# The high parts of q and k: two transfers on POOL's queue instead of two engine copies

## The reference

```python
scores = scale * np.matmul(q, k.transpose(0, 1, 3, 2))
cum = np.cumsum(np.maximum(s, 0.0), axis=-1)
bias = -(cum[:, :, :, None] - cum[:, :, None, :])
scores = np.where(causal, -1000000000.0, scores + np.minimum(bias, 0.0))
attn = softmax(scores)                       # with 1e-9 added to the sum
x = (attn @ v) with heads side by side       # 2304 x 512
x = np.maximum(np.maximum(x @ w1, x @ w2), x @ w3) @ w_out      # inner width 768
y = ((x @ w_a) * (x @ w_b)) @ w_out2                            # inner width 1536
```

## Time and profile before

| | us |
|---|---|
| median of 3 runs | 982.70 (982.25 to 982.79) |
| the profiled execution, device time | 982.89 |
| its span, first to last instruction | 981.1 |
| PE busy | 941.4 (96%) |
| weight loads busy | 859.0 (88%) |
| DVE busy | 465.4 (47%) |
| ACT busy | 406.4 (41%) |
| POOL busy | 215.7 (22%) |
| granted clock of TensorE over the span | 1.00 |

### The profile page before, as it was taken

The page is one execution under the profiler, slowest core; times in us unless marked ns, Lnnn a source line. Parts: engine busy times, 40 slices in busy tenths (PEclk is TensorE's granted clock), DMA queues, the critical chain, the costliest instruction groups (busy, mean ns, idle before and its releaser), DMA issues.

```text
span 981.1 us, 15222 instructions
## 1 busy us (share of the span) xinstructions
PE 941.4 (96%) x5776; PEld 859.0 (88%) x5776; DVE 465.4 (47%) x1054; ACT 406.4 (41%) x912; POOL 215.7 (22%) x309
## 2 busy tenths in 40 slices
PE   3789899999999999999999999999999999999998
PEld 2588899999999999999999888888888888888898
DVE  6789788877666577563233433221122112211212
ACT  4778677676655556543223432211121112111211
POOL 6868554453432423410000000000000000000000
PEclk9999999999999999999999999999999999999999
DMA  3644322222121221100032332200020001000100
GB/s 115 225 147 141 96 85 71 68 75 77 63 79 39 84 65 53 48 2 27 16 130 88 101 97 92 77 9 1 0 82 5 1 1 65 1 0 1 43 1 22
DMA packets 29240, 58.74 MB, mean 60 GB/s; under 512 B 3184, under 2 KB 15568, under 8 KB 29136
## 3 DMA queue, kind: packets, MB, share of 16 engines
q1 hardware_dynamic: 29168, 57.77, 18.4%
HBM read 47.82 MB, written 9.88 MB: 59 GB/s over the span
## 4 chain that ended last, share of the span: by engine, by line
PE 93%; issue 2%; DVE 1%; DMA 1%; ACT 1%; POOL 1%; SPq 0%; DVEq 0%; POOLq 0%; ACTq 0%
PE bank L1175 30%; PE bank L1047 23%; PE bank L1190 15%; PE bank L1067 8%; PE bank L998 6%; PE bank L1028 6%; PE bank L1014 5%; DMA qk_st<-cum_row 1%; DVE soft L790 0%; DMA qk_raw<-in_qk 0%; POOL soft L486 0%; ACT soft L536 0%; SPq L383 0%; DMA x_raw<-in_s 0%; POOL qk_st L477 0%
## 5 line engine op out<-in xcount | busy, mean ns | idle before, releaser
L957 DVE TENSOR_TENSOR g_raw<-bank,a_sb 128x512 f32<-128x512 f32 (+1 forms) x60 | 38.3, 638 | 298.5 <-PE bank L1175 298.5
L1047 PE MATMUL bank<-xs_hi,w_hi 128*128 128x256 f32 (+1 forms) x576 | 174.0, 302 | 1.9 <-DVE xs_lo L811 1.2
L1047 PE MATMUL bank<-xs_hi,w_lo 128*128 128x256 f32 (+1 forms) x576 | 170.7, 296 | 0.0
L1047 PE MATMUL bank<-xs_lo,w_hi 128*128 128x256 f32 (+1 forms) x576 | 170.6, 296 | 0.0
L486 POOL TENSOR_SCALAR soft<-soft,rden 128x576 f32<-128x576 f32 (+4 forms) x160 | 102.1, 657 | 216.6 <-DVE rden L776 216.6
L1175 PE MATMUL bank<-y_hi,w2b_hi 128*128 128x512 f32 (+1 forms) x360 | 132.4, 368 | 0.0
L1175 PE MATMUL bank<-y_lo,w2b_hi 128*128 128x512 f32 (+1 forms) x360 | 132.4, 368 | 0.0
L1175 PE MATMUL bank<-y_hi,w2b_lo 128*128 128x512 f32 (+1 forms) x360 | 132.4, 368 | 0.0
L1047 PEld LDWEIGHTS bank<-xs_hi,w_hi 128*128 128x128 f32 x576 | 109.4, 190 | 3.4 <-DVE xs_lo L811 1.4
L702 ACT ACTIVATE a_sb<-bank 128x512 f32<-128x512 f32 (+1 forms) x60 | 33.3, 555 | 188.5 <-PE bank L1175 188.5
L536 ACT ACTIVATE soft<-soft,neg_max 64x576 f32<-64x576 f32 (+4 forms) x160 | 96.0, 600 | 35.4 <-DVE neg_max L790 34.2
(11 more groups left out here) (84 smaller groups left out, 1825.7 us busy)
## 6 DMA issues: line engine op xcount, KB each, us to landing
qk_raw<-in_qk SPq DMA_DIRECT2D x32, 576.0 KB, 3.8
w_raw<-in_w SPq DMA_DIRECT2D x40, 384.0 KB, 3.6
v_raw<-in_v SPq DMA_DIRECT2D x32, 160.0 KB, 2.2
y_raw<-y_dram SPq DMA_DIRECT2D x4, 1024.0 KB, 5.5
outT<-o_stage SPq DMA_DIRECT2D x16, 256.0 KB, 2.1
qk_raw<-in_qk SPq DMA_DIRECT2D x8, 256.0 KB, 3.2
y_dram<-m_tmp SPq DMA_DIRECT2D x8, 160.0 KB, 1.8
y_dram<-h_raw SPq DMA_DIRECT2D x8, 160.0 KB, 1.8
```

Of the source, the lines that this page charges most:

```text
L1047: ins = nc.tensor.matmul(up_ps[g][:, 0:width1(c)], up1_w(w, f, g, kc), x[:, kc, 0:width1(c)], start=(kc == 0 and at == 0), stop=(kc == KC ...
```

## The change

POOL's copy `upper` and ACT's copy `lower` are removed with their semaphores. In the place of `upper` POOL's queue issues two transfers per job (`round_qk`), straight from the input in memory into `qk_st`: q and k for the upper half into blocks 0 and 1, and k and q for the lower half into blocks 1 and 2. The destination is float32r, so the transfer rounds. The two raise `qk_rounded[x % 2]` by 16 each. SP's load shrinks to the lower half, 64 partitions. `split_q` and `split_k` now wait for both the raw data and `qk_rounded`; the scores wait for `qk_rounded`. `round_qk(0)` and `round_qk(1)` stand at the very start of POOL's queue, ahead of the constants.

```diff
             def load_qk(x):
-                need(sp, upper_done, x - 1)
                 need(sp, qk_split, 2 * (x - 1))
-                dst, src = qk_raw[x % 2][:, :], qk[head(x), :, :]
+                dst, src = qk_raw[x % 2][DH:P, :], qk[head(x), DH:P, :]
...
         def _(pool):
+            def round_qk(x):
+
+                need(pool, score_done, TB[max(x - 1, 0)])
+                need(pool, qk_split, 2 * (x - 1))
+                cols = keys(x)
+                for p0, block in ((0, 0), (DH, 1)):
+                    nc.gpsimd.dma_start(qk_st[x % 2][p0:p0 + DH, block:block + 2, 0:cols],
+                                        qk[head(x), p0:p0 + DH, :].rearrange("p (a n) -> p a n", a=2)[:, :, 0:cols]
+                                        ).then_inc(qk_rounded[x % 2], 16)
+
+            round_qk(0)
+            round_qk(1)
             nc.gpsimd.memset(ones, 1.0).then_inc(ones_ready, 1)
...
-            upper(0)
-            upper(1)
...
                 if n != FIRST[0] - 1 and live(n + prepared(n)):
-                    upper(n + prepared(n))
+                    round_qk(n + prepared(n))
...
         def _(act):
-            def lower(x):
-
-                act.wait_ge(qk_loaded[x % 2], 16 * (x // 2 + 1))
-                need(act, score_done, TB[max(x - 1, 0)])
...
             def split_q(x):
-                dve.wait_ge(lower_done, x + 1)
+                dve.wait_ge(qk_loaded[x % 2], 16 * (x // 2 + 1))
+                dve.wait_ge(qk_rounded[x % 2], 32 * (x // 2 + 1))
...
                 if k == 0:
-                    pe.wait_ge(upper_done, n + 1)
+                    pe.wait_ge(qk_rounded[n % 2], 32 * (n // 2 + 1))
```

More of the change, by code:

```diff
@@ L270, in program @@
         v_loaded = sem("v_loaded")
-        upper_done, lower_done, qk_split = sem("upper_done"), sem("lower_done"), sem("qk_split")
+        qk_rounded = [sem("qk_rounded0"), sem("qk_rounded1")]
+        qk_split = sem("qk_split")
         v_hi_done, v_split = sem("v_hi_done"), sem("v_split")
@@ L470, in _ @@
                                     base=0, pattern=[[-1, P]], channel_multiplier=1).then_inc(ident_ready, 1)
[L472 to L479, removed]
             def normalise(n, k):
@@ L534, in exp @@
                 act.wait_ge(neg_done, TB[n] + k + 1)
+                if TB[n] + k == 0:
+                    act.wait_ge(init_done, 3)
                 i = tiles(n)[k]
@@ L578, in _ @@
             act.wait_ge(init_done, 1)
-            nc.scalar.activation(sums_eps[:, 0:1], sums[0][:, 0:1], ACT.Exp)
-            lower(0)
-            lower(1)
+            nc.scalar.activation(sums_eps[:, 0:1], sums[0][:, 0:1], ACT.Exp).then_inc(init_done, 1)
             def w1_hi_copy(piece):
@@ L596, in alone_slot @@
                 exp(n, 2)
-                if n < FIRST[0] - 1:
-                    lower(n + 2)
                 if ahead_of(n) is not None:
@@ L620, in sparse_slot @@
                     pt_hi_copy(m, 1)
-                lower(n + 1)
                 exp(n, 2)
@@ L645, in slot @@
                     x_hi(rest, KC - 1)
-                if live(n + 1):
-                    lower(n + 1)
                 if pending_row(n) is not None:
```

## The result

The changed kernel takes 1040.39 us in the median (1038.55 to 1043.68), the kernel before 982.75 us on the same chip: a ratio of 1.059 (95% interval 1.058 to 1.060), 58 us slower, where 23 us were forecast. The profiled execution took 1039.98 us, its span is 1038.2 us.

The account below looks back on a forecast made before the run. In sparse slots DVE's standstill at `split_q` was taken to be kernel time, while PE has a reserve in dense slots. Terms 12 + 5 + 2 + 4 = +23 us took 982.9 to 1006 us; 8-in-10 range 984 to 1040.

Parts of the forecast that it names:

- L: Time from POOL being free to issue until both transfers have landed; forecast 4.0 us, bounds 2.6 to 7.6 us.
- Sparse slots with w1 work: Jobs 10 to 16: DVE stalls at `split_q` where its lead is shorter than L, less some stretching; +12 us.
- Sparse slots without it: Jobs 17 to 25: leads mostly about 3.5 us, DVE stalls for the rest of L; +5.1 us.
- Dense slots: Jobs 26 to 39: shortfalls of 6.5 us, mostly covered by PE's reserve of about 0.5 us a slot; +2 us.
- Start and slots 1 to 8: Start effects cancel, then POOL's own pace of about 4.7 us a job costs 6 jobs x 0.6; +4 us.
- (b): Sign in the profile: 3.8 to 4.2 us from start of the first issue to landing of the second.
- (c): Sign: DVE idle ahead of `split_q` for a transfer into `qk_st`, 30 to 35 us in sum.
- (e): Sign at the start: first scores at about 10.8 us instead of 9.19.
- (f): Sign at the end: the last stretch, 554 us long, unchanged.
- Rival 1: Transfers hide behind the leads if L is 2.6 us or less; 981 or 979 us, not slower; chance 0.11.
- Rival 2: DVE starves POOL's transfers, L becomes 6 us; 1018 to 1065 us; chance 0.12 together with one other rival.
- Rival 3: PE leaves its upper clock level during stalls, six slots at half speed; about 1048 us; chance 0.03.

Follow-up runs that it names:

- the filler run: Changed kernel plus 24 needless products on PE ahead of `output(m)` in 12 sparse slots; 1047.52 us, ratio 1.066 to the kernel before.
- the best version: Changed kernel with jobs 0 to 9 by engine copies, jobs 10 to 39 by transfers issued early, behind `split_v(n)` for job n+2; 979.90 us, ratio 0.9974.

## Why the prediction was wrong, step by step

**What bounds the kernel** was read rightly: a stall of DVE at `split_q` comes out in the kernel's time, and reciprocal, normalise, transfers, split and reciprocal form one loop that doesn't heal. The direction, the place and the price of 20 to 25 us per microsecond of L held (24 between the lower half alone and the pair).

**L is the step that failed.** "A transfer of 144 KB lands like v's 160 KB." A half is 64 partitions of 1152 elements of 4 bytes, 288 KB; the size was halved by a slip, though the earlier trace rows give 576 KB for both halves. The 288 KB land 3.8 us after the start of their issue, not 1.0 + 1.85 = 2.85. The two are not side by side either: the second needs 4.5 us from its own start. The issue was over-priced: 0.59 and 0.53 us, not 1.0 each, and that took back 0.9 us. From the end of the second issue to its landing it is 4.0 us where 1.85 and 0.15 stood. So L = 5.1 in place of 4.0 us. The row that would have told was there: 576 KB in 3.8 us from SP's queue, and 3.8 + 1.0 us of issue is 4.8, which the prediction priced at about 1028 us.

The Trainium skill (DMA: Bandwidth & Descriptors, Rules for kernel authors) says that two transfers to disjoint halves of the partitions serialize and asks for one of 128. This trace agrees in part: the second lands 1.3 us after the first, more than the 0.6 us between their issues. The estimate of 992 us from the fit on that page was further off than the forecast; with 288 KB the fit gives an estimate of 2.7 us for a transfer, the trace shows 3.8.

**Sparse slots with w1 work**, jobs 10 to 16: +12 forecast, +19.0 measured. The seven jobs all had a lead below 4.0 us; 1.1 us more of L is 7 x 1.1 = 7.7, so the sum re-priced is 19.7.

**Sparse slots without it**, jobs 17 to 25: +5.1 forecast, +14.3 measured. Re-priced 5.1 + 9 x 1.1 = 15.0.

**Dense slots**: +2 forecast, +11.9 measured. Here too the mechanism held and L was the wrong term. At 5.1 us the leads of the 14 jobs fall short by 20.2 us in all, not by 6.5. The reserve that the prediction set against that, about 0.5 us a slot, is there. From the reciprocal to the next split the 14 slots take 22.2 us more than before. From the split to the reciprocal they take 10.3 us less, for in the kernel before DVE also waits in that stretch, for PE's scores and for ACT, and a DVE that comes late finds these ready. DVE behind the split of job 30, before and after:

```profile
286.55 0.76 DVE L790 CUSTOM_DVE_ANT_0 soft<-bank,causal 64x576 f32<-64x576 f32 x1 [1.63 <-PE bank L998]
```

```profile
337.30 0.76 DVE L780 CUSTOM_DVE_ANT_0 soft<-bank,causal 64x576 f32<-64x576 f32 x1
```

Where no such wait is left, the slot pays in full. That of job 28 takes 13.81 us in the kernel before, in the changed one 15.2:

```profile
280.18 2.78 POOL L490 TENSOR_SCALAR soft<-soft,rden 128x128 f32<-128x128 f32 x5 [9.92 <-DVE rden L766]
282.89 1.12 POOL L466 DMA_DIRECT2D qk_st<-in_qk  x2
...
295.44 2.78 POOL L490 TENSOR_SCALAR soft<-soft,rden 128x128 f32<-128x128 f32 x5 [9.96 <-DVE rden L766]
```

```profile
288.15 0.76 DVE L745 TENSOR_TENSOR qk_st<-qk_raw,qk_st 64x576 fp32r<-64x576 f32 x1 [2.52 <-DMA qk_st<-in_qk]
...
295.15 0.19 DVE L766 RECIPROCAL rden<-sums_eps 128x5 f32<-128x5 f32 x1 [0.16 <-DVE sums_eps L763]
```

From split to reciprocal DVE takes 7.0 us here in both kernels; from reciprocal to transfers issued and landed it is 0.3 + 2.7 + 5.1. That makes 15.2 with the hand-overs. Re-priced, the term is 20.2 less 14 x 0.5, 13.2 us.

**Start and slots 1 to 8**: +4 forecast, +12.4 measured. The first rows:

```profile
1.25 2.62 POOL L466 DMA_DIRECT2D qk_st<-in_qk  x4 [0.81 <-POOLq L1224]
3.86 0.60 POOL L472 MEMSET x_raw<- 32x576 f32 x1
...
11.06 1.19 PE L988 MATMUL bank<-qk_st 128*128 128x128 f32 x4 [11.06 <-DMA qk_st<-cum_row]
...
19.42 0.42 DVE L745 TENSOR_TENSOR qk_st<-qk_raw,qk_st 64x256 fp32r<-64x256 f32 x1 [5.48 <-DMA qk_st<-in_qk]
```

The memset slips to 3.86 us and the scan behind it by 0.8 us, not 1.5, but an instruction behind the scan took 1.54 us in place of 0.45, and so the first scores come at 11.06 us (10.8 forecast, 9.19 before). The rest is crowding, which the prediction had not priced. Around 13 to 19 us the DMA engines are nearly full, among other things with the cumulated sums and the first weights (their busy tenths from 10 to 24 us):

```profile
DMA  0000000017993789997999999410000597860000
```

The 128 KB transfers of job 2 take 5.1 and 6.2 us there; those of job 9, 288 KB each, take 6.3 and 7.8.

**The sum again.** With L at 5.1 the three stages from job 10 on come to 19.7 + 15.0 + 13.2 = 47.9 us, where 45.2 were measured and 19 forecast. With the +4 of the start that is 52 us in place of the 23 forecast, so L explains most of what was missing. The start lost 8.4 us more than its +4, the three stages 2.7 less than their re-priced sum: 57.6 in all.

**The checks named.** (a) 80 issues, but of 0.59 and 0.53 us, not 1.0. (b) 5.1, not 3.8 to 4.2 us. (c) DVE's idle time is at line 745 and put down to the transfer, but 76.1 us, not 30 to 35. (d) The slots of jobs 11 to 14 take 12.7 to 13.2 us, not 11.8 to 12.3. (e) Right to 0.3 us, with the luck told above. (f) Right: no loss behind attention.

**Rivals.** Rival 1 (the transfers hide) is what happens once they are issued early, from job 10 on. Rival 2 gave about the right time by a wrong mechanism: no issue is longer than 0.82 us, and in the best version, with DVE busy for 54.10 of 62 us, they take 0.52 to 0.60 us. Rival 3 did occur, and cost nothing that can be found. The granted clock was 0.50 in seven pieces between 76.7 and 230.3 us, 31 us in all (not eight and 37 as the expectation of the filler run has it), in the slots in which PE stands still; by stretch, and one group of weight loads in it:

```profile
76.80:79.90 3.10, 3.10 (x13) 2.91 (x13) 1.91 (x5) 0.97 (x3) 3.10 (x4) 0.50 0.14 50
```

```profile
L988 PEld LDWEIGHTS bank<-qk_st 128*128 128x128 f32 x4 | 1.2, 332 | 0.0
```

The argument against it, "the first 50 us with PE far emptier show 1.00 too", was unsound. In the kernel before, the weight loads of the scores took 324 ns in the mean up to 56 us, much as at the granted 0.50 above, the lower level of 1.2 GHz; later ones took 190 ns:

```profile
L998 PEld LDWEIGHTS bank<-qk_st 128*128 128x128 f32 x48 | 11.7, 324 | 18.9 <-issue 13.7 <-POOL qk_st L477 3.7 <-DVE neg_max L790 1.3
```

The trace's first record of the clock is at 56.1 us, so the 1.00 ahead of it stands for no record. The duration of a fixed piece of work tells the clock where the column doesn't.

**What stays open**: part of why the kernel without rounding is 6 us slower than the changed one, the 2.7 us of the larger scratch, how much of the start's loss each crowded transfer makes, and what of the 2.6 us of the best version comes from where.

## What to carry to other kernels

Replacing an engine's copy by a transfer trades work that nobody waited for against latency, so place the transfer a whole stage ahead of its reader, behind only what it truly needs, and keep it out of the stretch in which the DMA engines are already full. Before pricing a loop, list who is in it: each microsecond of latency inside counts up to once per round (22 us over 30 rounds here), and what covers it is only the time in which the loop already waits for others. Work out a transfer's bytes from shape times element size, and set them beside a row of the same size, before anything hangs on them.

## What the runs showed of the hardware

- An issue on POOL's queue of 64 partitions by two rows held POOL for 0.52 to 0.82 us, 0.59 us for the first of a pair and 0.53 for the second, and for 0.52 to 0.60 us where DVE was busy 54.10 of 62 us. With half the bytes it was no shorter, 0.67 and 0.58 us. So the row taken for it, a copy of as much data at 1.15 us, said nothing about it.
- From start of issue to landing: 2.5 us at best for 128 KB, 2.8 us for 144 KB, 3.8 us for 288 KB alone, at the start with the DMA engines nearly full 5.1 to 7.8 us for 128 and 288 KB, 4.5 us for the second of a pair.
- Rounding to float32r on the way cost nothing that shows: 3.8 and 4.6 us to landing without, 3.8 and 4.5 us with it.
- POOL's queue has a bound that no row names: with 1024 bytes of scratch for it the eighth transfer waited 3.67 us at its issue, with 2048 it didn't.
- A weight load of 128x128 from `qk_st` took 190 ns at a granted clock of 1.00 and 332 ns at 0.50.
